# Second stage's queries loaded ahead of its values, weight pieces split sooner, identity products in TensorE's pauses, two key tiles on GpSimd

## The reference

```python
def _attn_ref(q, k, v):                 # 8 batches, 8 heads, 576 tokens, 64 wide
    q_s = q - np.max(q, axis=-1, keepdims=True)
    q_s = np.exp(q_s)
    q_s = q_s / (np.sum(q_s, axis=-1, keepdims=True) + 1e-09)
    k_s = k - np.max(k, axis=2, keepdims=True)
    k_s = np.exp(k_s)
    k_s = k_s / (np.sum(k_s, axis=2, keepdims=True) + 1e-09)
    kv = np.einsum('bhsd,bhse->bhde', k_s, v)
    return np.einsum('bhsd,bhde->bhse', q_s, kv)
...
def _moe_ref(x, g_ln, w_ch1, w_ch2):    # 512 wide, hidden 2048
    mu = np.mean(x, axis=-1, keepdims=True)
    var = np.mean((x - mu) ** 2, axis=-1, keepdims=True)
    xn = (x - mu) / np.sqrt(var + 1e-06) * g_ln
    ch = np.maximum(xn @ w_ch1, 0.0) @ w_ch2
    return x + ch
...
```

## Time and profile before

| What | Value |
|---|---|
| median of 3 runs | 1351.04 us (1349.72 to 1351.27) |
| the profiled execution | 1352.02 us, its span 1350.0 us |
| TensorE busy | 1275.5 us, 94% of the span |
| DVE, ACT, POOL busy | 695.5, 462.7, 241.9 us |
| mean bandwidth | 65 GB/s |

### The profile page before, as it was taken

One profiled execution on the slowest core, in us unless ns is written; L12 is line 12 of the kernel. 1 busy time (PEld: TensorE's weight loads), 2 busy tenths in 40 slices (PEclk: granted clock), 3 DMA queues, 4 the chain that ended last, 5 costly groups with the idle time before them and its releaser, 6 DMA issues.

```text
span 1350.0 us, 19776 instructions
## 1 busy us (share of the span) xinstructions
PE 1275.5 (94%) x7312; PEld 1073.6 (80%) x7312; DVE 695.5 (52%) x1801; ACT 462.7 (34%) x1031; POOL 241.9 (18%) x264
## 2 busy tenths in 40 slices
PE   3679999999999999999999999996899999999986
PEld 3568888888888888888888888886788898888875
DVE  5636355455454464563553233115667766676652
ACT  3344131121121222212211111212566666666663
POOL 1322100000000000000000000113554544652321
PEclk9889999999999999999999999999799999999997
DMA  8452440531621612702701302303102102200111
GB/s 168 123 112 67 117 83 11 135 59 26 139 40 35 146 23 69 126 9 70 133 4 32 94 15 68 90 0 93 47 19 71 50 23 71 71 17 21 36 36 35
DMA packets 257228, 87.27 MB, mean 65 GB/s; under 512 B 200048, under 2 KB 245104, under 8 KB 257136
## 3 DMA queue, kind: packets, MB, share of 16 engines
q1 hardware_dynamic: 252448, 84.85, 26.9%
q10 hardware_dynamic: 4688, 1.18, 0.6%
HBM read 49.29 MB, written 19.92 MB: 51 GB/s over the span
## 4 chain that ended last, share of the span: by engine, by line
PE 88%; DVE 4%; issue 3%; ACT 1%; DMA 1%; POOL 1%; SPq 1%; ACTq 0%; POOLq 0%; DVEq 0%
PE hb L1284 29%; PE yb L1364 28%; PE sc L1284 15%; PE ob L1501 4%; PE tb L1483 4%; PE pa L1301 3%; PE sc L1470 3%; PE pa L1292 1%; DVE pt_lo L1245 1%; DMA vsb<-in_v_dram 1%; POOL prob L710 1%; ACT pt_hi L887 1%; DMA ksb<-in_k_dram 0%; DMA qx<-in_q_dram 0%; PE pa L1313 0%
## 5 line engine op out<-in xcount | busy, mean ns | idle before, releaser
L1084 DVE SCALAR_TENSOR_TENSOR hid_lo<-hb,hid_hi 128x512 fp32r<-128x512 f32 x144 | 99.6, 691 | 413.4 <-ACT hid_hi L781 413.4
L781 ACT ACTIVATE hid_hi<-hb 128x512 fp32r<-128x512 f32 x144 | 86.0, 598 | 636.7 <-PE hb L1284 636.1
L1364 PE MATMUL yb<-hid_hi,w_hi 128*128 128x512 f32 x576 | 230.2, 400 | 7.3 <-DVE hid_lo L1084 7.3
L1284 PE MATMUL hb<-xn_hi,w_hi 128*128 128x512 f32 x576 | 228.3, 396 | 0.0
L1364 PE MATMUL yb<-hid_hi,w_lo 128*128 128x512 f32 x576 | 225.4, 391 | 0.0
L1364 PE MATMUL yb<-hid_lo,w_hi 128*128 128x512 f32 x576 | 225.1, 391 | 0.0
L1284 PE MATMUL hb<-xn_lo,w_hi 128*128 128x512 f32 x576 | 224.5, 390 | 0.0
L1284 PE MATMUL hb<-xn_hi,w_lo 128*128 128x512 f32 x576 | 224.5, 390 | 0.0
L1364 PEld LDWEIGHTS yb<-hid_hi,w_hi 128*128 128x128 f32 x576 | 108.6, 189 | 31.2 <-DVE hid_lo L1084 7.4
L1284 PEld LDWEIGHTS hb<-xn_hi,w_hi 128*128 128x128 f32 x576 | 108.3, 188 | 25.5 <-issue 2.2
L1364 PEld LDWEIGHTS yb<-hid_lo,w_hi 128*128 128x128 f32 x576 | 108.8, 189 | 23.6 <-issue 1.7
(11 more groups left out here) (181 smaller groups left out, 2168.8 us busy)
## 6 DMA issues: line engine op xcount, KB each, us to landing
qx<-in_q_dram SPq DMA_DIRECT2D x32, 288.0 KB, 5.1
ksb<-in_k_dram SPq DMA_DIRECT2D x8, 1024.0 KB, 5.6
stage<-in_moe_w_ch_dram SPq DMA_DIRECT2D x16, 512.0 KB, 3.8
xn_lo<-ksb SPq DMA_DIRECT2D x128, 64.0 KB, 2.0
y_scratch<-ysb SPq DMA_DIRECT2D x32, 256.0 KB, 3.0
ysb<-xsb SPq DMA_DIRECT2D x128, 64.0 KB, 2.1
out_dram<-osb SPq DMA_DIRECT2D x32, 256.0 KB, 2.0
y_in<-y_scratch SPq DMA_DIRECT2D x28, 288.0 KB, 3.5
```

The source lines that it names most:

```text
L781: act.activation(HID[f % 2][0][:], hb[f % 2][:], ACT.Relu).then_inc(sems["hhi_a"], 1)
L1084: dve.scalar_tensor_tensor(out=lo[:], in0=hb[f % 2][:], scalar=0.0, in1=plain(hi[:]), op0=ALU.max, op1=ALU.subtract).then_inc(sems["hlo_v" ...
L1284: ins = pe.matmul(dst, l, r, start=(n == 0), stop=(n == len(terms) - 1))
L1364: ins = pe.matmul(yb[j][:], l, r, start=(f == 0 and m == 0 and not first), stop=(f == FT - 1 and m == 2), skip_group_check=True)
```

## The change

Five edits, all in the first stage, the first chunk, and the table of halves:

1. SP issues the queries of stage (0, 1) as soon as the first stage has read its own (`x_mm`), ahead of the tail's store, of pieces 8 and 9 and of the values; before, they stood behind the values.
2. ACT splits pieces 2 and 3 in the first stage, and each later pair one entry sooner (`PIECES_AT`); SP loads pieces 6 and 7 ahead of the second stage's keys.
3. TensorE gets 92 products of the identity with itself (`keep_clock`), 24, 6, 10, 12 and 40 of them at five places of the first stage. Nothing reads what they write.
4. In the first stage the key maximum is given a second time, to `hb`; ACT copies it to the new tile `ktop`, and GpSimd subtracts it from key tiles 3 and 4, which DVE did.
5. In `HALF`, the steps `kmaxT` to `qsub0` move one half later, for all stages that run beside an MLP.

```diff
-        HALF = dict(zip(ORDER, (3, 4, 5, 6, 7, 8, 9, 10, 11, 12, 13, 14,
+        HALF = dict(zip(ORDER, (3, 4, 6, 7, 8, 9, 10, 11, 11, 12, 13, 14,
                                 15, 16, 17, 18, 19, 20, 21, 22, 23, 29, 30)))
...
-        PIECES_AT = {0: [2, 3], 1: [4, 5], 3: [6, 7], 5: [8, 9], 7: [10, 11], 9: [12, 13], 11: [14, 15]}
+        PIECES_AT = {0: [4, 5], 1: [6, 7], 3: [8, 9], 5: [10, 11], 7: [12, 13], 9: [14, 15]}
...
                     load_v(st)
-                    load_q(st)
                     if not first:
+                        load_q(st)
                         move_tokens(c)
...
-            for n in range(EARLY - 2):
+            for n in range(EARLY):
                 load_piece(n)
             sp_.wait_ge(xn_t, CT)
             load_k((0, 1))
+            need(sp_, "x_mm", (0, 0), NT)
+            load_q((0, 1))
             store_tail((0, 0))
-            for n in range(EARLY - 2, EARLY):
-                load_piece(n)
...
+            pool.wait_ge(ktop_a, 1)
+            for t in (3, 4):
+                need(pool, "ksub_v", (0, 0), t)
+                top = ktop[0][0 : ROWS[t], :].rearrange("p (h d) -> p h d", h=H)
+                pool.tensor_tensor(k_tile(t), k_tile(t), top, ALU.subtract).then_inc(sems["ksub_v"], 1)
...
+            act.wait_ge(kmax_h, 1)
+            act.copy(ktop[0][:], hb[1][:]).then_inc(ktop_a, 1)
             for s in ("ksub0", "ksub1", "qsub0", "qsub1"):
                 step(s, START)
-            high_piece(0)
-            high_piece(1)
+            for n in range(4):
+                high_piece(n)
...
-                    for t in ((0, 1), (2, 3, 4))[int(s[4])]:
+                    for t in ((0, 1), (2,) if is_first(st) else (2, 3, 4))[int(s[4])]:
...
+            def keep_clock(n, dst):
+
+                for _ in range(n):
+                    pe.matmul(dst[:, 3 * P : 4 * P], ident[:], ident[:], start=True, stop=True)
+
...
             START = (0, 0)
+            keep_clock(24, yb[1])
             step("kmaxT", START)
+            keep_clock(6, yb[1])
             step("kbc", START)
+
+            pe.matmul(hb[1][:], ones[:], kmx[0][:], start=True, stop=True).then_inc(kmax_h, 1)
+            keep_clock(10, yb[1])
             pe.wait_ge(v_in, 16 * NT)
...
             ins.then_inc(sems["kv_mm"], 1)
+            keep_clock(12, yb[1])
             need(pe, "kv_v", START, 2)
...
+            need(pe, "x_v", START, 1)
+            keep_clock(40, yb[3])
```

More of the change, by code:

```diff
@@ L72, in program @@
         PW = 2
-        VS, kmx, XN, stage = [None, None], [None, None], [None, None], [None] * 4
+        VS, kmx, ktop, XN, stage = [None, None], [None, None], [None, None], [None, None], [None] * 4
         def v_and_xn(x):
@@ L78, in v_and_xn @@
                 kmx[x] = sb(f"kmx{x}", [P, D], F32, st)
+                ktop[x] = sb(f"ktop{x}", [P, D], F32, st)
             XN[x] = [sb(f"xn{x}_{part}", [P, KT, CW], F32R, st1) for part in ("hi", "lo")]
@@ L348, in program @@
         xn_t, x_t = sem("xn_t"), sem("x_t")
+        kmax_h, ktop_a = sem("kmax_h"), sem("ktop_a")
         xnT_v, xT_v, t_in, r_in = sem("xnT_v"), sem("xT_v"), sem("t_in"), sem("r_in")
@@ L1031, in step @@
                     need(dve, "qmx_v", st, 2)
+                    if is_first(st):
+                        dve.wait_ge(kmax_h, 1)
                     other = kmx[st[1]][:, 0 : HP * NG]
```

## The result

| What | Before | After |
|---|---|---|
| median | 1351.15 us (1349.72 to 1353.46, 4 runs) | 1339.18 us (1338.93 to 1339.40, 4 runs) |
| ratio of after to before, 95% interval | | 0.9903 [0.9890, 0.9916] |
| the profiled execution, and its span | 1352.02, 1350.0 us | 1339.03, 1337.1 us |

The kernel became 12.0 us (1.0%) faster; the forecast was 1337.9, with a range from 1334.8 to 1341.2. To see where it came from I cut each span at four events that every kernel has: the landing of the first queries (VectorE's first `qmx`), the first product of the first chunk (`hb<-xn_hi,w_hi`), the first token product of the second stage (`pa<-kv,qx`), and the moment at which TensorE runs dry ahead of the third block (its 3.28 us wait for `y_lo`).

The account below looks back on a forecast made before the run. TensorE, busy 1275.5 of 1350.0 us, bounds the kernel, so only its idle time can return. 10.4 + 1.9 + 2.5 - 1.7 = 13.1 off 1352.02 gives 1338.9, less 1.0 for the median: 1337.9, range 1334.8 to 1341.2.

Parts of the forecast that it names:

- A, the queries ahead: First chunk, block 5: earlier queries remove TensorE's 7.3 us wait for `hid_lo` and 3.1 of slow clock; gain 10.4.
- B, the key maximum: First chunk: TensorE reaches `kmaxT` half a block later, so 0.2 of its 2.1 us wait stays; gain 1.9.
- C, the first stage: Before the MLP: L989 comes 1.4 us earlier and identity products keep the clock up; `mlp1` starts at 45.45, gain 2.5.
- D, the new pause: Block 5: GpSimd's pieces delay the query maximum's last small step and the subtractions, so TensorE waits; loss 1.7 us.
- the rival: Block 5: the four copies of the query maximum wait for GpSimd too; loss 2.4 us, time 1338.6; chance 0.11.
- Waits do bite: Opposite rival: DVE's small steps slip in beside GpSimd, so gains total 16.2 us, time 1334.8; chance 0.15.
- the clock was held where it mattered: Opposite rival, first stage: identity products do not hold the clock, that stage gains nothing, time 1340.4; chance 0.14.
- the identity products ran at 1.2 GHz: Rival, first stage: identity products all run slow, the 40 end at 56 us; 3.4 slower, time 1354.4; chance 0.04.

Follow-up runs that it names:

- q_behind_v: The changed kernel with the second stage's queries issued behind its values again; median 1338.72 us, ratio to the kernel before 0.9907.
- before_q_early: The kernel before with only the earlier issue of the second stage's queries added; median 1342.84 us, ratio to the kernel before 0.9927.
- old_halves: The changed kernel with the `HALF` table of before, run twice; medians 1342.70 and 1340.90 us, ratio to the kernel before 0.9928 both times.
- qmax_sooner: The changed kernel with the query maximum one half sooner, rest of the new table kept; median 1338.36 us, ratio to the kernel before 0.9895.
- best_two: The changed kernel with the query maximum one half sooner and GpSimd's piece 3 after the first chunk's tokens are normalised; median 1338.24 us, ratio 0.9902.

## Why the prediction was right, and where its steps were off

**A, the queries ahead (forecast 10.4).** Its size held: 9.99 us with this edit alone, and no wait of TensorE for `hid_lo` is left. The step that failed is whose gain it is. The prediction gave it to edit 1, and in the same paragraph noted that piece 7 is now split at about 63, not 77. It did not follow this through: values at 63 put the queries behind them at 67, early enough by themselves. q_behind_v shows it: without edit 1 only 0.54 us are lost.

**B, the key maximum (1.9).** Right by size: TensorE comes to the maximum half a block later (63.74, forecast 63.75) and no longer waits, and with the old table the 2.1 us are back. The way was right in the main. The prediction let each of the four passes wait for one of GpSimd's instructions until 63.95; only two did so at length, as in the kernel before. The first took 0.94, and the third slipped in at 59.74, ahead of GpSimd's instruction at 59.87, and took 0.72. So they ended at 63.25, and nothing of the 2.1 us stayed where 0.2 was forecast. What the prediction missed is that the same edit acts in the later chunks. It read 79.99 busy of 80 us and said that nothing was to be had there. The 0.17 us per chunk does not show in that number, since each product of 512 columns is drawn 0.39 us long while the next one starts 0.23 after it. Missed: 1.28.

**C, the first stage (2.5).** Measured 2.41. The tile was taken over at 29.58 (forecast 28.85 to 29.9), and the first MLP product started at 45.50 (45.45). The prediction named the wrong step: L989 of before, the first with two inputs from SBUF, was to wait until 39.8. Held was the one ahead of it (L983 of before, L992 now), which has one, until 39.65; the step that was named began at 40.21 and was not held. So the normalisations began at 41.00, 0.4 later than the 40.6 of the forecast, and the way from there to the MLP took 4.50 us where 4.85 was forecast. That these two cancel is luck. So is part of the 2.41 itself: it is counted from an execution of before whose first stage took 28.89, and in before_q_early the same stage took 30.10. The 40 identity products hold the clock, as it said; the first 52 brought 0.35 us or nothing, because VectorE then runs into GpSimd. GpSimd's key tiles cost nothing, and what they bring (0.37) goes the same way.

**D, the new pause (-1.7).** Measured -1.46, the wait of TensorE ahead of the token products. The way to it was the rival's: the copies waited and the subtractions did not, and these ended 87.81 - 77.43 = 10.4 us behind the start of the maximum, where the rival said 10.5. The Trainium skill (Advanced Engine Details and Errata, GPSIMD Details) says that GpSimd conflicts with VectorE's instructions in a two-port mode as well as with those that have two SBUF inputs. This trace agrees in so far as the copies, which have one input, took 4.68 us beside GpSimd and 0.85 without it; that they run in such a mode no run here shows. The rival's price of 2.4 was too high by 0.9: behind the subtractions VectorE needed 6.4 us and not 6.9, and TensorE asked for the result 15.4 after the maximum's start and not 14.95. That the forecast's 1.7 lies nearer to 1.46 than the rival's 2.4 is luck: it let the maximum's last small step and the subtractions wait, and neither did.

**The sum.** The two profiled executions differ by 12.99 us, the forecast said 13.1. In it two things that I did not forecast nearly cancel: 1.28 in the chunks, and -1.52 behind them. The median came out 1.3 above the forecast for a third reason. I took off 1.0 because the profiled execution of before lay above its median, and that of after does not (1339.03, median 1339.18).

The other rivals fell. Waits do bite (L992, copies); the clock was held where it mattered; and the identity products ran at 1.2 GHz only up to about 15 us, so the 40 ended at 40.0 and not after 53.

**What stays open.** The last stretch, which no edit touches, took 433.66 to 438.60 us in fourteen profiled executions. Part of it lies in how long TensorE runs at the lower clock after the third block's pauses. By 20 us, in the changed kernel:

```profile
900.00:920.00 20.00, 15.38 (x98) 14.88 (x96) 8.83 (x28) 3.22 (x10) 0.77 (x1) 0.83 0.48 127
920.00:940.00 20.00, 12.38 (x83) 11.18 (x81) 12.06 (x36) 6.26 (x19) 10.35 (x10) 0.83 0.23 77
```

And in the kernel before, for 20 us from the start of the same first pause:

```profile
914.00:934.00 20.00, 15.38 (x106) 14.67 (x105) 9.37 (x30) 3.65 (x11) 1.52 (x2) 0.91 0.53 140
```

From the end of the first pause to the end of the second the changed kernel takes 12.88 us and the kernel before 11.63. Another part is the third pause, in which TensorE waits for VectorE's `nmax`: it lasted 8.58 to 9.12 us in the three executions with the longest last stretch (old_halves, qmax_sooner, best_two), and 7.28 to 7.76 in the other eleven. Whether all this follows from when the block starts, or is chance, no run here decides: the four runs of the changed kernel lie within 0.5 us, those of the kernel before within 3.7, and old_halves and its repetition, which are the same program, differ by 3.35 in this stretch.

## What to carry to other kernels

When two edits each take away the reason for the same wait, price each alone and the two together: here each was worth 10 us, and so were both. A busy share of 100% of an engine whose instructions overlap in the drawing does not say that it never waits; compare the distance from start to start at each step that needs another engine, and multiply by the chunks. And moving a step of VectorE off one GpSimd instruction may put it, or its follower, under the next; look at both neighbours before the table is changed.

## What the runs showed of the hardware

- VectorE waited for the end of GpSimd's running instruction in more cases than passes over two SBUF tiles: a step of 128x4 with constants (0.17 to 1.39 us), four copies of 32x72 (0.85 to 4.68, two of them held), four subtractions of 128x576 (2.76 to 7.15, two of them held), one small product of two tiles (0.16 to 2.06). Statistics (0.69 us), reciprocals (0.20), and steps that read a product's result (0.17 and 0.76) kept their lengths beside GpSimd's pieces in the first stage.
- GpSimd pays as well, when VectorE gets in between: two pieces took 4.70 us beside the four copies and 5.55 beside the four subtractions. A pass of the key maximum that began at 59.74, ahead of GpSimd's instruction at 59.87, took 0.72, and GpSimd's instruction 2.84, where it takes 2.35 in the first stage.
- In the first stage the 80 key products took 2.70 us when TensorE had been idle ahead of them for 1.6 to 2.5 us (three kernels with the 10 identity products before that pause), and 3.83 to 4.80 when it had been idle for 2.75 to 3.6 (six such kernels). Their first token tile came 10.56 us after the queries in the three, and 10.8 to 12.1 in the six. The idle time and the slower products go together in these nine executions; that the one is the cause of the other, no run shows.
